# Routing matmuls of a mixture-of-experts kernel: two passes over the one-hot matrices joined into one and moved, and the w2 pieces waited for one at a time

## What is computed

```python
attn = softmax(mask(q @ k.T / 8)) @ v            # window of 64 keys, 4 x 8 heads, 576 positions
x = ((attn @ w1) * (attn @ w2)) @ w3 @ w_out      # the kernel folds w3 @ w_out into W
logits = x @ w_gate;  e = argmax(logits)          # 8 experts, each row goes to one
scale = softmax(logits)[e] * sigmoid(x @ w_output_gate)[e]
out[row] = scale * (relu(x[row] @ ew1[e]) @ ew2[e])
```

## Time and profile before

| | us |
|---|---|
| median of 3 runs (718.04 to 718.18) | 718.11 |
| the profiled execution | 717.64 |
| its span, first to last instruction | 715.9 |

### The profile page before, as it was taken

How to read it: one execution, slowest core, us unless ns; L and a number is a source line. 1 busy time by engine, 2 the same in 40 slices (tenths; PEclk the granted TensorE clock), 3 DMA queues, 4 the chain that set the end, 5 groups by cost and what they waited for, 6 DMA issues and landing times.

```text
span 715.9 us, 15038 instructions
## 1 busy us (share of the span) xinstructions
PE 707.6 (99%) x5153; PEld 646.0 (90%) x5154; DVE 321.6 (45%) x596; ACT 295.3 (41%) x697; POOL 125.9 (18%) x191
## 2 busy tenths in 40 slices
PE   9999999999999999999999999999999999999997
PEld 7998999999999999999999999888888888888885
DVE  4667555312145425441222568845456554662221
ACT  4667455322045526442211153444446444552121
POOL 6132011100021011110000001222222122222211
PEclk9999999999999999999999999999999999999999
DMA  9876121320012152114301033756265754511110
GB/s 304 286 248 190 60 67 38 119 74 1 16 53 60 47 159 61 32 46 156 124 1 45 1 101 135 269 179 217 71 223 189 234 171 135 182 35 44 32 44 30
DMA packets 48062, 80.13 MB, mean 112 GB/s; under 512 B 5325, under 2 KB 29901, under 8 KB 48016
## 3 DMA queue, kind: packets, MB, share of 16 engines
q1 hardware_dynamic: 42976, 64.01, 27.7%
q0 software_dynamic: 5040, 15.47, 6.3%
HBM read 70.03 MB, written 10.49 MB: 112 GB/s over the span
## 4 chain that ended last, share of the span: by engine, by line
PE 98%; DVE 2%; issue 0%; POOLq 0%; ACT 0%; ACTq 0%; DVEq 0%
PE bank L473 28%; PE bank L475 27%; PE bank L474 27%; PE bank L566 3%; PE bank L537 3%; PE bank L720 3%; PE bank L553 2%; PE bank L698 1%; PE bank L521 1%; PE bank L497 1%; PE bank L514 1%; PE bank L499 1%; PE bank L501 1%; PE bank L680 1%; DVE w3l L1003 0%; DVE nmx L985 0%
## 5 line engine op out<-in xcount | busy, mean ns | idle before, releaser
L473 PE MATMUL bank<-Wh,abh 128*128 128x272 f32 (+1 forms) x288 | 83.5, 290 | 0.0
L475 PE MATMUL bank<-Wh,abl 128*128 128x272 f32 (+1 forms) x288 | 82.0, 285 | 0.0
L474 PE MATMUL bank<-Wl,abh 128*128 128x272 f32 (+1 forms) x288 | 81.8, 284 | 0.0
L1068 DVE TENSOR_TENSOR wbuf<-raw,wbuf 128x1024 f32 (+1 forms) x64 | 75.3, 1221 | 12.7 <-ACT wbuf L851 12.6
L1385 POOL TENSOR_TENSOR prob<-prob,rec 128x384 f32<-128x384 f32 x48 | 43.8, 934 | 179.3 <-DVE rec L993 179.3
L1266 DVE TENSOR_TENSOR hTl<-bank,hTh 128x512 fp32r<-128x512 f32 x44 | 28.4, 685 | 95.6 <-ACT hTh L909 95.6
L473 PE MATMUL bank<-wbuf,hTh 128*128 (+1 forms) x176 | 70.7, 402 | 0.0
L473 PE MATMUL bank<-wbuf,xsTh 128*128 (+1 forms) x176 | 70.4, 400 | 0.0
L781 ACT ACTIVATE prob<-prob,nmx 128x128 f32<-128x128 f32 x144 | 55.9, 390 | 32.5 <-DVE nmx L985 32.5
L475 PE MATMUL bank<-wbuf,hTl 128*128 (+1 forms) x176 | 68.8, 391 | 0.0
L475 PE MATMUL bank<-wbuf,xsTl 128*128 (+1 forms) x176 | 68.6, 390 | 0.0
(11 more groups left out here) (202 smaller groups left out, 1453.0 us busy)
## 6 DMA issues: line engine op xcount, KB each, us to landing
raw<-in_expert_w SPq DMA_DIRECT2D x64, 512.0 KB, 4.5
qT<-in_qT SPq DMA_DIRECT2D x24, 192.0 KB, 3.2
kT<-in_kT SPq DMA_DIRECT2D x24, 192.0 KB, 3.5
x_rows<-x_sb POOLq DMA_DIRECT2D x18, 256.0 KB, 2.3
w3r<-in_w3T SPq DMA_DIRECT2D x8, 512.0 KB, 5.3
wo<-in_w_out SPq DMA_DIRECT2D x8, 256.0 KB, 6.7
woT<-in_w_outT SPq DMA_DIRECT2D x4, 512.0 KB, 7.4
vA<-in_v SPq DMA_DIRECT2D x16, 128.0 KB, 2.1
```

The lines of the kernel that those rows point to most:

```text
L473: pe.matmul(dst, lh, rh, start=first, stop=False)
L474: pe.matmul(dst, lh, rl, start=False, stop=False)
L475: return pe.matmul(dst, ll, rh, start=False, stop=last)
L1068: dve.tensor_tensor(wbuf[:, bass.ds(wcol(e, part, 1, c * PC), PC)], raw[part * NP1 + c][:, :], f32(wbuf[:, bass.ds(wcol(e, part, 0, c * PC ...
```

## The change

`ids` and `scales` become one tensor `values` with four sets of 26 columns for each tile, finished at step 39 of the routing chain. TensorE multiplies each `R[t]` once, by 104 columns, into bank 6. This pass stands behind the first four transposes of slot 0 and no longer inside hidden(0) and behind each four transposes. VectorE doesn't wait for it behind the routing chain: it splits pieces 5 and 6, writes the first half of `hTl`, then waits for the pass, works out `gid` and `ssc`, splits piece 7 and writes the second half of `hTl`. In slot 0 `project` waits for the w2 pieces one by one, at f = 0, 2, 4 and 6. `x_transposes(1)` goes from behind f = 3 to behind f = 4.

```diff
-        ids, scales = put("ids", NT * 2 * NSLOT, F32R), put("scales", NT * 2 * NSLOT, F32R)
+        values = put("values", NT * 4 * NSLOT, F32R)
...
-            def routed(dst, values, tiles):
-                for t in tiles:
-                    mm = pe.matmul(dst[:, 0:2 * NSLOT], R[t][:, :], values[:, t * 2 * NSLOT:(t + 1) * 2 * NSLOT],
-                                   start=(t == 0), stop=(t == NT - 1))
-                return mm
-
-            def slot_ids():
-                pe.wait_ge(rt, RT_IDS)
-                pe.wait_ge(rt_R, NT - ET)
-                routed(bank[6], ids, range(NT)).then_inc(rt_Ru, 1)
-
-            def slot_scales(half):
-                pe.wait_ge(rt, RT_SCALES)
-                mm = routed(bank[7], scales, range(half * (NT // 2), (half + 1) * (NT // 2)))
-                if half:
+            def slot_values(n):
+                if n == 0:
+                    pe.wait_ge(rt, RT_VALUES)
+                    pe.wait_ge(rt_R, NT - ET)
+                    for t in range(NT):
+                        mm = pe.matmul(bank[6][:, 0:4 * NSLOT], R[t][:, :], values[:, t * 4 * NSLOT:(t + 1) * 4 * NSLOT],
+                                       start=(t == 0), stop=(t == NT - 1))
                     mm.then_inc(rt_Ru, 1)
...
-            def project(s, e, tail, between=None):
+            def project(s, e, tail, between=None, first=False):
                 last = tail // 2
-                pe.wait_ge(ew_lo[1], (e + 1) * NP1)
+                if not first:
+                    pe.wait_ge(ew_lo[1], (e + 1) * NP1)
                 if not last:
                     pe.wait_ge(y_ok, s + 1)
                 for f in range(KF):
                     if f % 4 == 0:
                         pe.wait_ge(hT_lo, s * 2 + (f // 4 + 1))
+                    if first and f % 2 == 0:
+                        pe.wait_ge(ew_lo[1], f // 2 + 1)
...
             def second_slot(f):
-                if f == KF // 2 - 1:
+                if f == KF // 2:
                     x_transposes(1)
...
-            hidden(0, 0, slot_ids)
+            hidden(0, 0)
             pe.wait_ge(xA_ok, NT + 1)
-            h_transposes(0, slot_scales)
-            project(0, 0, 0, second_slot)
+            h_transposes(0, slot_values)
+            project(0, 0, 0, second_slot, True)
...
-            dve.wait_ge(rt_Ru, 1)
-            then(dve.tensor_scalar(id1[:, :], bank[6][:, 0:NSLOT], float(P), None, ALU.mult))
-            then(dve.tensor_tensor(id1[:, :], id1[:, :], bank[6][:, NSLOT:2 * NSLOT], ALU.add))
-            then(dve.tensor_scalar(gid[:, 0:NSLOT], id1[:, :], -float(P), 0.0, ALU.add, ALU.max))
-            dve.sem_inc(idx_ok, 1)
...
+            def first_half_out():
+                hT_half(0, 0)
+                dve.wait_ge(rt_Ru, 1)
+                then(dve.tensor_scalar(id1[:, :], bank[6][:, 0:NSLOT], float(P), None, ALU.mult))
+                then(dve.tensor_tensor(id1[:, :], id1[:, :], bank[6][:, NSLOT:2 * NSLOT], ALU.add))
+                then(dve.tensor_scalar(gid[:, 0:NSLOT], id1[:, :], -float(P), 0.0, ALU.add, ALU.max))
+                dve.sem_inc(idx_ok, 1)
+                then(dve.tensor_copy(ssc_hi[:, :], bank[6][:, 2 * NSLOT:3 * NSLOT]))
+                then(dve.tensor_tensor(ssc[:, :], ssc_hi[:, :], bank[6][:, 3 * NSLOT:4 * NSLOT], ALU.add))
+                dve.sem_inc(scale_ok, 1)
 
             for p in range(2 * CT - 1, 2 * NP1):
+                if p == 2 * NP1 - 1:
+                    first_half_out()
                 split_lo(0, p // NP1, p % NP1)
-            hT_out(0)
-            dve.wait_ge(rt_Ru, 2)
-            then(dve.tensor_copy(ssc_hi[:, :], bank[7][:, 0:NSLOT]))
-            then(dve.tensor_tensor(ssc[:, :], ssc_hi[:, :], bank[7][:, NSLOT:2 * NSLOT], ALU.add))
-            dve.sem_inc(scale_ok, 1)
+            hT_half(0, 1)
```

More of the change, by code:

```diff
@@ L1232, in _, with in_slot @@
             then(dve.tensor_tensor(sohv, over(first_row, NSLOT), under(thr, NT), ALU.is_equal))
-            def in_slot(t, w):
-                return t[:, :].rearrange("p (t w s) -> p t w s", w=2, s=NSLOT)[:, :, w, :]
+            def in_slot(w):
+                return values[:, :].rearrange("p (t w s) -> p t w s", w=4, s=NSLOT)[:, :, w, :]
             for w in range(2):
-                then(dve.tensor_tensor(in_slot(ids, w), sohv,
+                then(dve.tensor_tensor(in_slot(w), sohv,
                                        tok[:, w * NT:(w + 1) * NT].unsqueeze(2).broadcast_to([P, NT, NSLOT]), ALU.mult))
-            assert step[0] == RT_IDS, step[0]
             dve.wait_ge(rt_act, 2)
@@ L1248, in _ @@
             then(dve.tensor_tensor(scll[:, :], scl[:, :], f32(sclh[:, :]), ALU.subtract))
-            then(dve.tensor_tensor(in_slot(scales, 0), sohv, f32(sclh[:, :]).unsqueeze(2).broadcast_to([P, NT, NSLOT]), ALU.mult))
-            then(dve.tensor_tensor(in_slot(scales, 1), sohv, over(scll, NSLOT), ALU.mult))
-            assert step[0] == RT_SCALES, step[0]
-            dve.wait_ge(rt_Ru, 1)
-            then(dve.tensor_scalar(id1[:, :], bank[6][:, 0:NSLOT], float(P), None, ALU.mult))
-            then(dve.tensor_tensor(id1[:, :], id1[:, :], bank[6][:, NSLOT:2 * NSLOT], ALU.add))
-            then(dve.tensor_scalar(gid[:, 0:NSLOT], id1[:, :], -float(P), 0.0, ALU.add, ALU.max))
-            dve.sem_inc(idx_ok, 1)
+            then(dve.tensor_tensor(in_slot(2), sohv, f32(sclh[:, :]).unsqueeze(2).broadcast_to([P, NT, NSLOT]), ALU.mult))
+            then(dve.tensor_tensor(in_slot(3), sohv, over(scll, NSLOT), ALU.mult))
+            assert step[0] == RT_VALUES, step[0]
             def relu(s):
@@ L1260, in relu, with hT_half @@
                 dve.tensor_scalar(h_sb[:, 512:FF], bank[2][:, :], 0.0, None, ALU.max).then_inc(h_okD, 1)
+            def hT_half(s, n, last=0):
+                cols = slice(n * 512, (n + 1) * 512)
+                dve.wait_ge(hT_hi, s * 2 + (n + 1))
+                dve.tensor_tensor(hTl[last][:, cols], bank[3 + n][:, :], f32(hTh[last][:, cols]), ALU.subtract).then_inc(hT_lo, 1)
             def hT_out(s, last=0):
                 for n in range(2):
-                    cols = slice(n * 512, (n + 1) * 512)
-                    dve.wait_ge(hT_hi, s * 2 + (n + 1))
-                    dve.tensor_tensor(hTl[last][:, cols], bank[3 + n][:, :], f32(hTh[last][:, cols]), ALU.subtract).then_inc(hT_lo, 1)
+                    hT_half(s, n, last)
+            def first_half_out():
[8 more added lines that the diff above has]
+                dve.sem_inc(scale_ok, 1)
             for p in range(2 * CT - 1, 2 * NP1):
+                if p == 2 * NP1 - 1:
+                    first_half_out()
                 split_lo(0, p // NP1, p % NP1)
-            hT_out(0)
-            dve.wait_ge(rt_Ru, 2)
-            then(dve.tensor_copy(ssc_hi[:, :], bank[7][:, 0:NSLOT]))
-            then(dve.tensor_tensor(ssc[:, :], ssc_hi[:, :], bank[7][:, NSLOT:2 * NSLOT], ALU.add))
-            dve.sem_inc(scale_ok, 1)
+            hT_half(0, 1)
             then(dve.tensor_scalar(pad[:, :], id1[:, :], 0.0, float(OOB), ALU.is_equal, ALU.mult))
@@ L1455 @@
 RT_Z = 8
-RT_IDS = 31
-RT_SCALES = 39
+RT_VALUES = 39
 def kernel(**inputs):
```

## The result

The changed kernel took 721.04 us (median of 6 runs, 720.41 to 722.82) against 718.08 us before (6 runs), a ratio of 1.0041 with a 95% interval of 1.0030 to 1.0052. The forecast was 718.1 us and no change; the range ended at 719.5. The profiled execution took 721.25 us, its span was 719.3 us.

The account below looks back on a forecast made before the run. TensorE was taken as the bound: 2.05 us won, given back as 0.2 us at f = 4, some 1.55 at the gather and 0.2 at xsTl. 717.64 - 0.05 + 0.47 gave 718.1 us; range 717.5 to 719.5.

Parts of the forecast that it names:

- parts 1 and 2: TensorE up to project(0): 18 joined matmuls replace 36, saving 2.05 us; inputs arrive in time except at f = 4.
- the stall of 0.2 us before f = 4: In project(0), TensorE waits until 449.05 us for the second half of hTl.
- rival E: Routing matmuls: 104 columns cost four times as much, 173 ns each; +1.2 us, 719.3 us; chance 0.03.
- The start of the gather: GpSimd starts the second slot's gather at 447.33 us, since gid is written 3.1 us later.
- the 2.05 us to hidden(1, 0): From the start of x_transposes(1) to hidden(1, 0), which waits for xsTl: 2.05 us with the hand-over.
- The 2 us won on TensorE: Fewer routing matmuls shrink TensorE's own work by 2.05 us, given back almost in full at f = 4, gather and xsTl.
- the term L of part 3: Time from the second slot's gather start to its landing: 3.9 us, ends 3.4 and 5.3; shift of hidden(1, 0) is L - 3.95.
- my argument that the traffic was now spread: Pieces 5 and 6 are freed 0.9 us earlier, so their reloads are mostly through when the second slot's gather moves.
- upper end of 5.3 us: Upper end for the gather's landing time, taken from the gather before, which landed with reloads of pieces 5 to 7 queued.
- rival F: TensorE's idle 1.5 us lowers its clock and hidden(1, 0) runs at half speed: 5.4 us more, about 723.5; chance 0.02.
- the forecast idle of 1.5 us: TensorE's wait for the second slot's gather before x_transposes(1), about 1.5 us.
- Rival C: Reloads of piece 7 and the rest of piece 6 delay the gather, L 4.5 to 5.5: 718.7 to 719.7 us; chance 0.20.

Follow-up runs that it names:

- e2: Changed kernel with VectorE writing the second half of hTl before it splits piece 7; 719.02 us, ratio 1.0019 to the kernel before.
- e3: Changed kernel with SyncE holding piece 7's reload for expert 1 until the second slot's gather has landed; 719.74 us, ratio 1.0020 to before.
- e1: Changed kernel with x_transposes(1) behind f = 6 instead of f = 4, nothing else; 721.85 us, ratio 1.0048 to before.
- e4: Changed kernel with the edits of e2 and e3 together; 719.90 us, ratio 1.0015 to before.
- e6: As e4, with piece 6's reload also held until the second slot's gather has landed; 718.51 us, ratio 1.0001 to before.
- e5: Changed kernel with two passes again: ids early inside hidden(0), scales in one pass behind the first four transposes; 719.02 us, ratio 1.0010 to before.
- b1: Changed kernel, joined pass behind nine of twelve matmuls of hidden(0)'s second half, then transposes; VectorE does ids, scales, both hTl halves, piece 7; 719.55 us.
- c0: The kernel before, unchanged, measured once more; 717.94 us, ratio 0.9994 to before.
- b2: As b1, but with the first four transposes ahead of the joined pass and VectorE's list laid out anew; 718.68 us, ratio 1.0008 to before.
- b3: As b2, with xsTl of the third slot written before the last split of w2's first piece; 717.34 us, ratio 0.9986 to before.

## Why the prediction was wrong

**Right: where the time would go.** By its own steps: parts 1 and 2 are right within 0.1 us, the stall of 0.2 us before f = 4 among them; the rival E is out (18 matmuls of 104 columns in 2.03 us, 113 ns each). The start of the gather and its becoming what TensorE waits for were right too, and the 2.05 us to hidden(1, 0) were 0.11 short at the full clock (e2: 453.56 - 451.40 = 2.16). The 2 us won on TensorE were there and were given back, as forecast.

**Wrong: the term L of part 3.** I put 3.9 us with 3.4 and 5.3 as ends; it was 6.1. Two things stood behind it. The gather's instruction waited 0.96 us for VectorE's split of piece 7, which the change had put right in front of it; e2 shows this. And it then shared the DMA engines with the reload of piece 7, 1.8 us by e3's profile (1.2 against e1's); the two hang together, since without the wait the gather's data started ahead of that reload (e2); my argument that the traffic was now spread was right for pieces 5 and 6 only as long as the gather was 1 us late (e4, e6). The first of these stood in the trace before: gather(1)'s instruction took 1.44 us and gather(2)'s 1.03, and I took the landings without asking why. So the upper end of 5.3 us wasn't one: that landing had 0.4 us of waiting for a split in it, and the change could make it more.

**Wrong: rival F, the clock, at a chance of 0.02 and a price of 5.4 us.** I read from the earlier trace rows that TensorE could idle 2.6 us at the full clock, and set the forecast idle of 1.5 us against it. The idle stretch became 3.46 us because of L, and the clock fell: 3.18 - 2.16 = 1.02 us on top. It wasn't 5.4, since the clock was back at 1.00 by 456.5, before hidden(1, 0) started. And the bound was no bound: in e4 it fell after 1.96 us of idling, in e1 after two times 1.5. The sum closes: from hidden(0) to x_transposes(1) 15.71 us, 2.11 more than the 13.60 forecast, then 0.11 for the short 2.05 and 1.02 us of clock, is 3.24; forecast -0.05, measured 18.89 - 15.70 = 3.19. The rule of the Trainium skill that I had named beside F ("TensorE: Matmul & The Clock Gate", HAM oscillation: waits for DMA between groups of matmuls let the clock fall, and the work behind runs cold) is what the windows show for one such wait.

Rival C was the nearest to what happened. Its L ended at 5.5 and its time at 719.7 us because it had the traffic alone, and nothing for the clock. The forecast time hung on L: the 2 us won and the lateness of the gather came out as worked out.

## What to carry to other kernels

Where TensorE is the bound and has no idle time, the work removed is the small part of the question: find the longest chain that hangs on the moved step (here arithmetic, gather, transposes, split) and price it with what each engine does beside it at the new time. In this kernel a gather by GpSimd wants to start at a moment in which VectorE runs no split and no large reload is in the queues. Reordering adds no instruction, but it can make something else late (e5, b1). And a wait of TensorE costs more than its length once the clock falls, here 1.0 us on 3.46.

## What the runs showed of the hardware that I had not expected

- A GpSimd gather that starts during a VectorE subtraction with both inputs in SBUF (128 x 1024) is held until that ends: 1.99 us (after, e1, e3), 1.43 or 1.44 us (before, c0, e5) and 1.28 us (b2's loop), against 1.02 to 1.10 us without one; beside one that reads PSUM it isn't held (e2, e4, e6, b1: 1.07 us). A split that starts while the gather's instruction runs isn't slowed (e2: 1.22 us).
- The clock fell after idle stretches of 1.96 us (e4) and two of 1.5 us (e1), and stayed up after 1.62 (e3), 1.80 (e2) and 1.04 us (e6) in the profiled executions. In e1 it was at 0.50 to 461 us, 6 us after TensorE was busy again.
- Two delays of one DMA, the late instruction and the traffic, were worth 2.0 and 1.3 us by the medians when taken away one at a time, and together 1.2 us (e4; by the ratios 1.6, 1.5 and 1.9): not the sum. What the gather meets depends on when its instruction is done; with both reloads held L was 3.4 us (e6).
- Open: why the time outside the span varies in most versions with the joined pass (1.7 to 2.9 us for b3, 1.7 to 3.0 for e2), and not in before and e1 (1.7 to 1.9), and how long TensorE may idle before the clock falls in a given execution.
